# Unread products of ones ahead of the tensor engine's waits in a prologue: thirty in eight places instead of four in one

## The reference, cut to what matters

```python
def _attn_ref(q, k, v):                      # 4 batches, 8 heads, 576 rows, head size 64
    scores = scale * np.matmul(q, k.transpose(0, 1, 3, 2))
    rel = pos[:, None] - pos[None, :]
    mask_local = (rel >= 0) & (rel < 32)                                  # heads 0 to 3
    mask_strided = (rel >= 0) & (pos[None, :] % 32 == pos[:, None] % 32)  # heads 4 to 7
    attn = softmax(np.where(mask, scores, -1e9))
    return np.matmul(attn, v)

def reference(**inputs):
    x = attn_out.transpose(0, 2, 1, 3).reshape(2304, 512)
    h = x @ w_in                                   # 512 -> 2048
    x = where(h >= 1, h, where(h <= -1, 0, (h + 1) ** 2 / 4)) @ w_out     # 2048 -> 512
    # then a layer of 8 experts for the rows with x @ w_skip > 0; the others pass through
```

## Time and profile before

| | us |
|---|---|
| median of 3 runs | 511.61 (511.3 to 512.32) |
| the profiled execution | 512.21 |
| its span, first to last instruction | 510.4 |
| TensorE busy in the span | 498.2 (98%) |
| the prologue, to the first product of the first layer | 31.86 |
| mean granted clock over the span | 0.982 |

### The profile page before, as it was taken

How to read it: one execution, slowest core, us unless ns; L and a number is a source line. 1 busy time by engine, 2 the same in 40 slices (tenths; PEclk the granted TensorE clock), 3 DMA queues, 4 the chain that set the end, 5 groups by cost and what they waited for, 6 DMA issues and landing times.

```text
span 510.4 us, 8844 instructions
## 1 busy us (share of the span) xinstructions
PE 498.2 (98%) x3397; PEld 432.6 (85%) x3397; DVE 260.4 (51%) x594; ACT 195.4 (38%) x435; POOL 213.1 (42%) x235
## 2 busy tenths in 40 slices
PE   7898999899999999999999999999999999999996
PEld 5687888788998888888888888888998899888895
DVE  4957566753335536667633677662435252322322
ACT  4966566443223334335342434442322222322222
POOL 0559867673223235455533446552222322222221
PEclk9669999999999999999999999999999999999999
DMA  8993202100201203121210420100210008740001
GB/s 251 339 385 113 94 2 80 53 2 19 106 0 49 71 24 128 44 80 33 97 28 19 172 80 3 31 2 12 77 55 0 2 7 323 286 168 0 2 2 65
DMA packets 18977, 42.15 MB, mean 83 GB/s; under 512 B 2054, under 2 KB 3920, under 8 KB 18932
## 3 DMA queue, kind: packets, MB, share of 16 engines
q1 hardware_dynamic: 18836, 41.54, 23.8%
q0 software_dynamic: 96, 0.02, 0.0%
HBM read 32.94 MB, written 8.78 MB: 82 GB/s over the span
## 4 chain that ended last, share of the span: by engine, by line
PE 90%; DVE 6%; ACT 1%; issue 1%; DMA 1%; SPq 0%; POOL 0%; DVEq 0%
PE bank L1040 38%; PE bank L1024 38%; PE bank L863 4%; PE bank L827 4%; PE bank L844 3%; DVE row_sum L1185 1%; DMA qk<-in_qk_dram 1%; PE bank L967 1%; PE bank L948 1%; DVE prob_first L1159 1%; DVE bank L1168 1%; DVE prob L1175 1%; DVE row_max L1163 1%; DVE row_max L1173 1%; DVE row_sum L1188 0%
## 5 line engine op out<-in xcount | busy, mean ns | idle before, releaser
L1775 POOL TENSOR_TENSOR g_lo<-act_f,g_hi 128x384 fp32r<-128x384 f32 x96 | 97.4, 1014 | 196.9 <-ACT g_hi L1672 196.4
L1663 ACT ACTIVATE act_f<-act_f,half_col 128x384 f32<-128x384 f32 x96 | 59.1, 616 | 203.0 <-DVE act_f L1406 203.0
L1406 DVE TENSOR_SCALAR act_f<-bank 128x384 f32<-128x384 f32 x96 | 53.2, 554 | 144.9 <-PE bank L1024 136.7
L1024 PE MATMUL bank<-x_hi,win_hi 128*128 128x384 f32 x384 | 88.3, 349 | 0.6 <-DVE act_f L1409 0.6
L1040 PE MATMUL bank<-wout_hi,g_hi 128*128 128x512 f32 x285 | 85.1, 407 | 0.0
L1024 PE MATMUL bank<-x_hi,win_lo 128*128 128x384 f32 x384 | 84.4, 338 | 0.0
L1672 ACT CAST g_hi<-act_f 128x384 fp32r<-128x384 f32 x96 | 49.2, 512 | 91.6 <-DVE act_f L1409 91.4
L1024 PE MATMUL bank<-x_lo,win_hi 128*128 128x384 f32 x384 | 83.4, 335 | 0.0
L1040 PE MATMUL bank<-wout_hi,g_lo 128*128 128x512 f32 x285 | 81.0, 392 | 0.0
L1040 PE MATMUL bank<-wout_lo,g_hi 128*128 128x512 f32 x285 | 81.0, 392 | 0.0
L1024 PEld LDWEIGHTS bank<-x_hi,win_hi 128*128 128x128 f32 x384 | 67.0, 189 | 8.5 <-issue 1.5
(11 more groups left out here) (129 smaller groups left out, 430.9 us busy)
## 6 DMA issues: line engine op xcount, KB each, us to landing
w_early<-in_w_dram SPq DMA_DIRECT2D x4, 2048.0 KB, 9.0
qk<-in_qk_dram SPq DMA_DIRECT2D x12, 592.0 KB, 4.7
out_dram<-y_rows SPq DMA_DIRECT2D x18, 256.0 KB, 2.6
win_raw<-in_w_in_dram SPq DMA_DIRECT2D x16, 256.0 KB, 9.2
wout_raw<-in_w_out_dram SPq DMA_DIRECT2D x16, 256.0 KB, 9.5
y_dram<-y_rows SPq DMA_DIRECT2D x15, 256.0 KB, 2.8
v<-in_v_dram SPq DMA_DIRECT2D x6, 384.0 KB
v<-in_v_dram SPq DMA_DIRECT2D x6, 288.0 KB
```

What stands on the lines that cost most here:

```text
L1024: mm = pe.matmul(h_ps[s % 2][:, 0:CH], w[:, f, P * k:P * (k + 1)], x[:, k, cols], start=(at == 0), stop=(at == len(order) - 1))
L1406: dve.tensor_scalar(tile, h_ps[s % 2][:, 0:CH], -1.0, 1.0, ALU.max, ALU.min).then_inc(clip_ready, 1)
L1663: act.activation(tile, tile, ACT.Square, bias=half_col[:, 0:1], scale=0.5).then_inc(square_ready, 1)
L1775: pool.tensor_tensor(g_lo[:, s % RING, :], act_f[:, s % 2, :], g_hi[:, s % RING, :].bitcast(F32), ALU.subtract).then_inc(g_lo_ready, 1)
```

## The change

The number of unread products is now read from a table by step and unit. They stand ahead of the wait for the step's data and behind the wait for its bank. For S the two waits for banks are now ahead of the wait for the queries and keys. All other engines and queues keep their instructions and order.

```diff
+FILLERS = {("P", 0): 4, ("S", 1): 4, ("S", 2): 9, ("P", 2): 5, ("P", 3): 2, ("P", 4): 2, ("P", 5): 2, ("V", 4): 2}

             def scores(n):
                 u = UNITS[n]
+                take_bank(pe, "S", n, 0)
+                take_bank(pe, "S", n, 1)
+                warm_up(bank_of("S", n, 0), FILLERS.get(("S", n), 0))
                 if u.b == 0 and n < N_PRO:
                     pe.wait_ge(qk_loaded[u.p], 16 if strided(u.p) else 32)
...
-                take_bank(pe, "S", n, 0)
-                take_bank(pe, "S", n, 1)

             def transpose_probs(n):
...
                     take_bank(pe, "P", n, hh)
-                    if n == 0 and hh == 0:
-                        warm_up(bank_of("P", n, hh), 4)
+                    if hh == 0:
+                        warm_up(bank_of("P", n, hh), FILLERS.get(("P", n), 0))
                     pe.wait_ge(prob_ready, 2 * n + hh + 1)

             def values_of(n):
...
                 take_bank(pe, "V", n)
+                warm_up(bank_of("V", n), FILLERS.get(("V", n), 0))
                 for hh in range(2):
                     wait_free(pe, "P", n, hh)
```

## The result

| | before | changed |
|---|---|---|
| median of 7 runs, us | 511.30 (510.44 to 512.32) | 508.49 (508.14 to 510.03) |
| ratio, 95% interval | | 0.9958 (0.9944 to 0.9972) |
| profiled execution, its span, us | 512.21, 510.4 | 509.94, 508.1 |
| mean granted clock of the profiled execution | 0.982 | 0.993 |

A second set of six runs of the changed kernel gave 508.70 (507.98 to 509.80), ratio 0.9944 (0.9928 to 0.9961). The 13 runs of the two sets form groups by their mean clock: three with 0.998 to 1.000 at 508.0 to 508.5, six with 0.996 or 0.997 at 508.4 to 509.1, four with 0.993 at 509.8 to 510.0. None is near 515.

A forecast was written before the change was run, and what follows sets the result against it. It took TensorE, 98% busy, as the bound, its prologue clock low. Unread products before P2 (+1.0) and the other eight (+3.3), less 0.4 for an earlier rise, gave +3.9 us: 515.5 on the median's scale, range 507.8 to 516.8.

The forecast's parts named there:

- the early rise: Prologue, by the time S1 runs: four unread products before S1 leave no gap, so the clock rises at 5 to 8 us.
- the free nine before S2: Nine unread products before S2 take 2.07 us at full clock; S2 starts 0.8 later than its load allows, price nothing.
- the fall between 16.5 and 19.5: Between P0 and V0 the change adds no products, so the clock falls again between 16.5 and 19.5 us.
- the five ending at 22.4: Before P2, five unread products at 0.417 us each end at 22.4, so P2 starts 1.0 us later than before.
- A: Rival, chance 0.20: the clock never falls from 8 us on, first layer starts at 29.5, gain 3.8 at most, 507.8 us.
- B: Rival, chance 0.20: the clock falls, but V0 and the five before P2 bring it back; gain taken as 2.2, 509.4 us.
- With the clock low they stand on the path: The thirteen unread products from P2 to V4 delay the first layer from 31.9 to 36.2 us: +1.0 and +3.3.
- what is recorded as busy is not what counts here: At 18 to 31.9 us, half the busy time is transposes, taken not to count as activity, so the clock stayed low.
- The price where the clock does stay low: From P2 to the first layer: +1.0 + 3.3 - 0.4 = +3.9 us, with 0.417 us per unread product.
- VectorE's 0.64 us: S1 ends at or before 9.36, where VectorE took it up after 0.64 us idle; VectorE gains at most these 0.64.

The follow-up runs named there:

- the filled hole: The changed kernel with nine more unread products: one before P0's first half, two before its second, four and two before P1's halves; 508.37 us, ratio 0.9943.
- the early thirteen alone: The changed kernel without its unread products from P2 on, keeping those before S1 (4), S2 (9) and P0 (4); 511.80 us, ratio 1.0008.
- none: The changed kernel with no unread products but the six at the start; 511.72 us, ratio 1.0009.
- the eight alone: The changed kernel without the five before P2, all its other unread products kept; median 514.50 us, ratio 1.0034, eight of twelve runs at 514.2 to 515.6.

## Why the prediction was wrong

**Right:** the early rise in the profiled run, the free nine before S2 (VectorE took up unit 1's mask at 8.64 instead of 9.36, and M2 did not wait), the fall between 16.5 and 19.5 for want of products between P0 and V0 (the filled hole shows the cause), the five ending at 22.4, and rivals A and B as mechanisms. The rise was in part luck: in the profiled runs of the early thirteen alone (S0 in 1.12 us) and of none (S0 in 1.29, S1 in 1.12) the clock was up before any unread product ahead of S1 could act. With the four ahead of it S1 took 1.12 in all fifteen profiled runs; without them it took 2.02, 1.78 and 1.12. Three of thirteen runs of the changed kernel went as A by their mean clock, the others as B. A's 507.8 was 0.2 to 0.7 too low, B's 509.4 is near the middle of its runs.

**The step that failed:** "With the clock low they stand on the path", and ahead of it "what is recorded as busy is not what counts here: half of that time is transposes, the rest value products". From the stretch of 18 to 31.9 us before, I concluded that work of this kind, and with it V0 and five products behind it, would not raise the clock, and gave 0.20 to the case that it does (rival B). The stretch held one more difference, which TensorE's order shows as 72x72 at P2: the units from there on are strided, and their transposes and values use 72 rows. V0, V1 and the ones use 128, and V1 stands alone between strided work. In the profiled runs 8.7 us of products of 64 or 72 rows left the clock at 0.50; with ten transposes of 128 rows behind V0 it was back 1.7 us after their start. What the runs showed in place of the step: behind V0 and the five the clock came back at 23.8, the first layer started at 30.82 and not at 36.2, and none of thirteen runs was low.

**The price where the clock does stay low** was about 1 us short. With the eight alone it was 3.3 us over before, for 2.3. All thirty at a low clock, as forecast, are nearest in the three low runs with five of 72 by 72 or of 64 rows: 516.15, 516.16 and 517.63, 4.9 us or more over before (511.24), for 3.9. No trace of such a run was taken, and where the rest goes is open.

**Mis-sized in B:** the first layer started at 30.82, not at 30.1. I let ScalarE be the bound, with the times of before, and took unread products at full rate as nearly free. ScalarE waited for P2, which came 1.0 later: C2 started at 23.14 instead of 22.27, behind 1.48 us of idle time, and was still 0.9 late at H2 (27.73 instead of 26.84). But it was not the bound: the chain of waits of the changed kernel stays on TensorE from V0 to the first layer, but for 0.09 us, and the eight unread products stand in it with 2.05 us. Some of its pieces:

```profile
20.37 2.25 PE bank L812 x5
22.62 0.96 PE bank L848 x8
...
24.54 0.54 PE bank L812 x2
...
29.65 1.24 PE bank L868 x32
```

ScalarE's two rows:

```profile
23.14 0.88 ACT L1567 COPY prob_t<-bank 72x288 f32<-72x288 f32 x2 [1.48 <-PE bank L848]
...
27.73 0.68 ACT L1575 CAST x_hi<-bank 128x288 fp32r<-128x288 f32 x1
```

**VectorE's 0.64 us:** they arrived (8.64 for 9.36) and were worth nothing alone: 511.80 with the early thirteen only.

**Open:** what the clock does in the minority of runs in which small tiles were not followed by a low clock, and with it whether small tiles only fail to raise it or also let it fall; why the same program falls into different groups from run to run; and what the scores count for, which use 64 rows a head with the two heads in different halves of the array. No run here shows these.

## What to carry to other kernels

Filling TensorE's waits pays where its clock is low and it is itself on the path: here 2.8 us of 511, all of it from the thirteen from P2 on. With the five of them ahead of P2 none of thirteen runs was low, without them eight of twelve, and the other eight held the clock; the thirteen before S1 and S2 added nothing that these runs can tell. The busy share did not tell a stretch that stayed at 1.2 GHz from one behind which the clock rose (2.00 of 2.00 us in both). The rows that its products used did, so an unread product of all 128 partitions is the one to try first. Look at the times and clocks of single runs: a median over two groups (509.0 and 514.7 without the five) names a time that no kernel has.

## What the hardware showed

- 20 products of 64 rows by 128 columns, back to back for 8.71 us at 100% busy: granted clock 0.50 all through in the profiled run. 5 of 128 rows by 64 columns, behind V0: back at 1.00 by 24 us; 5 of 72 by 72 at the same place: back at 26.9. Ten fp32 transposes of 128 by 128: back at about 21.3, 1.7 us behind their start.
- Granted clock without the thirteen early ones: up before 6 us in two profiled runs (S0 in 1.12 and 1.29 us), not in a third (2.03).
- The printed clock of 1.00 before its first recorded change is not a measurement: in the kernel before, products there are 0.417 us apart, against 0.23 at full clock.
- An unread 512-column product costs 0.44 us at 1.2 GHz (8.75 / 20, drain included) and 0.22 at 2.4 GHz (4.48 us for twenty with 64 columns).
